# A three-stage kernel on one core: the TensorE order of the attention rounds, and two results in other PSUM banks

## What is computed

```python
for t in range(S):
    state = alpha[:, :, t, :, None] * state + np.einsum('bhd,bhe->bhde', k[:, :, t], v[:, :, t])
    y[:, :, t] = np.einsum('bhd,bhde->bhe', q[:, :, t], state)
```

## Time and profile before

| | us |
|---|---|
| median of 3 runs | 916.24 |
| lowest and highest | 914.87, 918.62 |
| the profiled execution, its own time | 919.07 |
| its span in the profile | 917.5 |
| PE busy | 881.7 (96% of the span) |
| DVE, ACT, POOL busy | 435.9, 320.4, 272.0 |
| attention rounds 0 to 15 | from 15.07 to about 187 of the span |

### The profile page before, as it was taken

How to read it: one execution, slowest core, us unless ns; L and a number is a source line. 1 busy time by engine, 2 the same in 40 slices (tenths; PEclk the granted TensorE clock), 3 DMA queues, 4 the chain that set the end, 5 groups by cost and what they waited for, 6 DMA issues and landing times. The chain is left out here.

```text
span 917.5 us, 16303 instructions
## 1 busy us (share of the span) xinstructions
PE 881.7 (96%) x5729; PEld 775.3 (85%) x5729; DVE 435.9 (48%) x826; ACT 320.4 (35%) x708; POOL 272.0 (30%) x279
## 2 busy tenths in 40 slices
PE   7999999888999999999998999999999999999995
PEld 5777787667899898998987899999999989999994
DVE  7777778782322223222234545445445445445442
ACT  4465646452322223222232233223223323223221
POOL 3113344545547544735807301001001001001001
PEclk9999999999999999999999999999999999999998
DMA  9886875768876897766806301001001002000000
GB/s 149 142 131 115 160 131 108 242 237 265 253 249 194 287 294 251 218 205 182 231 27 179 97 1 53 18 1 61 10 1 64 6 0 70 1 1 35 1 1 34
DMA packets 140975, 107.92 MB, mean 118 GB/s; under 512 B 103354, under 2 KB 129074, under 8 KB 140898
## 3 DMA queue, kind: packets, MB, share of 16 engines
q0 software_dynamic: 25696, 66.09, 22.9%
q1 hardware_dynamic: 115202, 40.79, 21.1%
HBM read 89.51 MB, written 17.35 MB: 116 GB/s over the span
## 5 line engine op out<-in xcount | busy, mean ns | idle before, releaser
L1396 POOL DMA_INDIRECT out<-of,idi x24 | 23.6, 983 | 370.2 <-DVE of L1482 305.5
L1216 PE MATMUL bank<-WX,hdTh 128*128 (+1 forms) x496 | 129.0, 341 | 3.6 <-issue 2.6
L1440 PE MATMUL bank<-xT_h,wi_h 128*128 128x512 f32 x288 | 114.1, 396 | 0.0
L1440 PE MATMUL bank<-xT_l,wi_h 128*128 128x512 f32 x288 | 113.6, 394 | 0.0
L1440 PE MATMUL bank<-xT_h,wi_l 128*128 128x512 f32 x288 | 113.4, 394 | 0.0
L1522 DVE TENSOR_SCALAR em<-ee 128x512 f32<-128x512 f32 x96 | 44.5, 464 | 136.3 <-ACT ee L1500 134.1
L1500 ACT ACTIVATE ee<-bank 128x512 f32<-128x512 f32 x96 | 57.3, 597 | 147.3 <-PE bank L1440 136.5
L1202 PE MATMUL bank<-WX,xdTh 128*128 (+1 forms) x372 | 99.7, 403 | 2.4 <-ACT xdTh L1242 1.3
L1503 ACT ACTIVATE g_h<-gg 128x512 fp32r<-128x512 f32 x96 | 60.6, 631 | 116.1 <-DVE gg L1527 114.4
L1140 POOL TENSOR_TENSOR WX<-raw_w,WX 128x3072 fp32r<-128x3072 f32 x14 | 95.6, 6829 | 17.6 <-DMA WX<-moe_w 13.2
L1531 DVE TENSOR_TENSOR g_l<-gg,g_h 128x512 fp32r<-128x512 f32 x96 | 69.7, 726 | 60.2 <-ACT g_h L1503 56.5
(11 more groups left out here) (212 smaller groups left out, 1392.8 us busy)
## 6 DMA issues: line engine op xcount, KB each, us to landing
WX<-moe_w POOLq DMA_DIRECT2D x14, 1536.0 KB, 10.1
raw_w<-moe_w POOLq DMA_DIRECT2D x14, 1536.0 KB, 7.8
xd<-sorted_x SPq DMA_DIRECT2D x31, 193.0 KB, 5.4
sorted_y<-yd SPq DMA_DIRECT2D x31, 192.5 KB, 4.0
xg<-sorted_y SPq DMA_DIRECT2D x6, 770.0 KB, 4.4
nat_a<-alpha SPq DMA_DIRECT2D x32, 144.0 KB, 3.2
nat_k<-k SPq DMA_DIRECT2D x32, 144.0 KB
nat_q<-q SPq DMA_DIRECT2D x32, 144.0 KB
```

Of the source, the lines that this page charges most:

```text
L1216: last = pe.matmul(y_out(t)[:, 0:DM], hdT[a][:, k * P:(k + 1) * P], WX[:, bass.ds(off + (b * WE + KD * F + k * DM), DM)], start=(k == 0 an ...
L1440: last = pe.matmul(bank[4 + i % 2][:, :], a[:, k, w], b[:, k, :], start=(k == 0 and m == 0), stop=(k == KD - 1 and m == 2))
```

## The change

In PE's table, `Yi0`, `Yi1`, `Ys0`, `Ys1` now stand together at the end of the round, so that both halves' logits with values run in one stretch and both halves' states with queries in the next. The transposes `Ta0`, `Ta1`, `Tq0`, `Tq1`, `Tk0` move ahead and are interleaved with `YN0` and `YN1`. To allow this, the second half of y goes to bank 6 instead of bank 7, and the increments of `KV` go to bank 5 instead of bank 6. So `YN0` now waits for `St5`, where it waited for `Kt1`. ACT's table changes with it: `yT0` and `yT1` are at the head of the next round around `Kt0`, and `Ea0` and `C1` come ahead of `Yn0`. `Rw` of the router, `Gq` of the last but one batch and one `SP` square move a few places, because bank 6 and the table changed.

```diff
-        ROUND_PE = (("KT0", 0), ("A0", 0), ("KT1", 0), ("Tk1", 1), ("KV", 0), ("A1", 0), ("YN0", -1), ("Ta0", 2), ("Yi0", 0),
-                    ("YN1", -1), ("Ta1", 2), ("Ys0", 0), ("Tq0", 1), ("Tq1", 1), ("Tk0", 2), ("Yi1", 0), ("Ys1", 0))
+        ROUND_PE = (("KT0", 0), ("A0", 0), ("KT1", 0), ("Tk1", 1), ("KV", 0), ("A1", 0), ("Ta0", 2), ("YN0", -1), ("Ta1", 2),
+                    ("Tq0", 1), ("YN1", -1), ("Tq1", 1), ("Tk0", 2), ("Yi0", 0), ("Yi1", 0), ("Ys0", 0), ("Ys1", 0))
-        ROUND_AC = (("yT1", -1), ("Kt0", 0), ("Kt1", 0), ("St1", 0), ("St2", 0), ("St3", 0), ("St4", 0), ("St5", 0),
-                    ("Yn0", -1), ("Ln0", -1), ("C1", 0), ("Ea0", 2), ("Yn1", -1), ("Ln1", -1), ("Ea1", 2), ("yT0", 0))
+        ROUND_AC = (("yT0", -1), ("Kt0", 0), ("yT1", -1), ("Kt1", 0), ("St1", 0), ("St2", 0), ("St3", 0), ("St4", 0), ("St5", 0),
+                    ("Ea0", 2), ("C1", 0), ("Yn0", -1), ("Ln0", -1), ("Ea1", 2), ("Yn1", -1), ("Ln1", -1))
...
         def y_bank(n, i):
-            return bank[1 if n == PAIRS - 1 and i else 7]
+            return bank[(1 if n == PAIRS - 1 else 6) if i else 7]
...
                             at_ = c % HC * P + DP * h
-                            last = pe.matmul(bank[6][DP * h:DP * h + DP, c * D:(c + 1) * D], ktsb[c // HC][:, at_:at_ + DP],
+                            last = pe.matmul(bank[5][DP * h:DP * h + DP, c * D:(c + 1) * D], ktsb[c // HC][:, at_:at_ + DP],
...
-                        acA.wait(pe, f"yT{1 - i}", n - 1 + i)
+                        acA.wait(pe, f"yT{i}", n - 1)
+                    for b in range(PARTIAL):
+                        if n == round_of(b, 1) and i:
+                            veA.wait(pe, "Rw", b)
...
-                        acA.wait(pe, "Kt1", n + 1)
+                        acA.wait(pe, "St5", n + 1)
...
-                    return ac.activation((st if i > 1 else std)[u][:, i, :], bank[6][:, (i - 1) * D:i * D], ACT.Copy,
+                    return ac.activation((st if i > 1 else std)[u][:, i, :], bank[5][:, (i - 1) * D:i * D], ACT.Copy,
```

More of the change, by code:

```diff
@@ L290, in build @@
                 {"R": ("Rp", "Rr"), "S5": ("Ng", "Nk"), "LA": ("Ns", "Nt", "Nr")})
-        SOON = ({"LA": ("Rl", "Rx", "Dl")}, {"R": ("Rc", "Rb", "Ro"), "F": ("Rs", "Rn", "Rd", "Y0"),
+        SOON = ({"LA": ("Rl", "Rx", "Dl")}, {"R": ("Rc", "Rb", "Ro"), "F": ("Rs", "Rn", "Rw", "Rd", "Y0"),
                                              "LA": ("Ng", "Nk", "Y1", "Y2", "Y3", "Y4", "Y5", "Y6", "Y7"),
-                                             "Qh1": ("Rw", "Rp", "Rr", "Ns", "Nt", "Nr")})
+                                             "Qh1": ("Rp", "Rr", "Ns", "Nt", "Nr")})
         LAST = ({"LA": ("Rl", "Rx", "Dl", "N0", "Rc", "Rb", "Ro", "Rs", "Rn", "Rd", "Rw", "Rp", "Rr", "Rz", "Ng", "Nk", "Ns", "Nt", "Nr",
@@ L297, in build @@
         ROUTE_PE = [({}, {"Ta0": ("CT",)})] * (BATCHES - 1) + [({"YN1": ("CT",)},)]
-        ROUTE_AC = [({}, {}, {"Ln0": ("Gq",)})] * (BATCHES - 2) + [({}, {"yT0": ("Gq",)}), ({"Ln1": ("SL", "Wc", "Gq")},)]
+        ROUTE_AC = [({}, {}, {"Ln0": ("Gq",)})] * (BATCHES - 2) + [({}, {"Ln1": ("Gq",)}), ({"Ln1": ("SL", "Wc", "Gq")},)]
         ROUTE_PO = [({"Zm": ("ID",)},)] * BATCHES
@@ L350, in steps_ac @@
                 i = place_of(out_, "St5") + 1
-                out_.insert(i, ("SP", PARTIAL * C + 2))
-                out_ += [("SM", PARTIAL)] + [("SP", PARTIAL * C + j) for j in range(3, C)]
+                out_[i:i] = [("SP", PARTIAL * C + j) for j in range(2, 4)]
+                out_ += [("SM", PARTIAL)] + [("SP", PARTIAL * C + j) for j in range(4, C)]
             for b, r in batches_of(n):
@@ L622, in step @@
                     acA.wait(pe, "St5", n - 1)
-                    for b in range(BATCHES):
-                        if n == round_of(b, 2):
-                            veA.wait(pe, "Rw", b)
                     for c in range(C - 1):
@@ L677, in step @@
                     veA.wait(pe, "Ro", n)
-                    acA.wait(pe, "St5", round_of(n, 1) if n < PARTIAL else PAIRS - 1)
+                    acA.wait(pe, "yT1", round_of(n, 0) if n < PARTIAL else PAIRS - 2)
                     for x, lhsT in enumerate((before, ones)):
```

## The result

The median went from 915.97 us (913.05 to 918.62) to 917.93 us (916.62 to 919.86), with 20 runs of each: a ratio of 1.0023, 95% interval 1.0013 to 1.0034, about +2 us. Forecast were +2.7 and "within 0.5%", and this is what came. The terms that make it up are not those of the forecast, though: that they add up to the right total is luck. The profiled execution of the changed kernel took 917.66 us (span 916.1).

What follows compares the result with a forecast made beforehand. PE was taken to set the pace of stage one. Terms -0.5 + 0.7 + 0.4 - 0.5 + 2.9 - 0.6 + 0.3 = +2.7 us on 916.2 gave 918.9 us; range from nearly 912 up to 923.5.

Steps and rivals of the forecast that it cites:

- Term 1: PE in each round: fewer changes of tiling, 0.64 us less work, 9 us over 14 full rounds if nothing waits.
- Term 2: Quiet rounds: YN1 waits 0.52 us for ACT's Ln0; round 10.19 against 10.31; rounds 2, 3, 4, 10 together -0.5.
- Term 3: Squares ahead of Yn0 on ACT delay YN1: +0.70 us in round 5, +0.4 in round 9; round 13 about -0.5.
- the formula: For rounds other than quiet ones: change in length equals the shift of YN1's start minus 0.38 us.
- Term 4: Late PE signals while POOL scatters: rounds 7, 8, 11, 12 +2.9 us, earlier scatters -0.6, rounds 14 and 15 +0.3.
- The clause on the bank: YN0's wait for St5, through a bank shared by address, costs nothing in quiet rounds, 2.2 us of standing in round 8.
- Round 6: ACT's table load now stands ahead of Ea1, for which Tk0 waits: 0 change, within 0.5 us.
- the scatter rounds pay little: Rival: late signals are out before St5 is wanted, four scatter rounds +0.1 each; about +0.8, 917 us; chance 0.20.
- the switches in full: Rival: Ln0 in time, each of 14 rounds gains PE's 0.64 us; -9, 907 us; chance 0.14.

Runs made afterwards that it cites:

- experiment 3: Changed kernel with ACT's Yn0 and Ln0 ahead of C1 and the two squares of rounds 5 and 9 at the round's end; 913.35 us, ratio 0.9956.
- experiment 5: Changed kernel with its last four PE steps ordered Yi0, Ys0, Yi1, Ys1, two more changes of tiling per round; 931.6 us, ratio 1.0089.
- experiment 6: Changed kernel with only ACT's Yn0 and Ln0 moved ahead of C1; 926.41 us, ratio 1.0051 to the kernel before.
- the kernel before, again: The kernel before, unedited, in a second execution under the profiler; 917.72 us.
- experiment 10: The kernel before with six matmuls of no use ahead of round 0, keeping PE busy; 915.01 us, ratio 0.9995; its profiled execution 914.59 us.
- experiment 7: Changed kernel with only the two squares of rounds 5 and 9 moved to the end of ACT's round; 924.67 us, ratio 1.0030.
- experiment 8: Changed kernel with the KV increments back in bank 6, so YN0 waits for Kt1, not St5; 926.25 us, ratio 1.0048.
- experiment 11: Changed kernel with Yn0, Ln0 ahead of C1 except round 14, squares at the end, Gq after Ln1, six matmuls ahead of round 0; 912.42 us, ratio 0.9969.
- experiment 4: Changed kernel with twelve matmuls nobody reads, six ahead of round 0 and six after the last YN1; 917.34 us, ratio 1.0004.

## Why the prediction was right, and where it was not

- **Term 1, mis-sized.** 0.64 us less PE work per round was forecast; the rows of experiment 3 give 0.44. I took `YN` for 0.67 where it follows transposes, without its 0.10 of coming in, since both use the whole array. It takes 0.75 (50.91 to 51.66) and 0.78 (52.40 to 53.18), together 0.19 too little. All other parts were right to 0.01 or 0.02 once the two short waits are taken out. So what costs is not the tiling alone; going from transposes to multiplying costs nearly as much with the tiling unchanged. Going back from `YN` to transposes costs nothing: the three of `Ta1` take 0.33 (52.19 to 52.52 in the changed kernel). Where the tiling did change, the price of 0.13 held (experiment 5). The Trainium skill (TensorEngine Tiling, Key Properties) speaks of changing the mode; this trace has a price between transposes and multiplying in one tiling too, 0.08 to 0.11 us on the way in.
- **Term 2, right in kind.** The wait is there for the reason given, at the time given (`YN1` at 6.13, forecast 6.09) and of nearly the size given (0.48 by starts, forecast 0.52), and it eats the whole gain. The round is 10.32 instead of 10.19 because `YN1` starts 0.04 later than forecast and takes 0.77 instead of 0.67. Experiments 3 and 6 confirm it: with `Yn0` ahead of `C1` quiet rounds are 10.09, 0.22 under the kernel before, and the rest of the 0.44 stays in the two short waits.
- **Term 3, right in kind, too small.** +0.95 in round 5 (forecast +0.70) and +0.95 in round 9 (forecast +0.4). `YN1` came at 7.27, where 7.28 was forecast. But the formula subtracted 0.38 for the work after it, and by rows that is 0.11 here (4.48 before, 4.37 after: 75.11 to 79.48) and 0.28 in a quiet round (4.20). So the step that was mis-sized is this 0.38. And the kernel before, again, has 10.69 in both rounds: the late mask of round 9 belonged to the first profile. Round 13 was forecast at -0.5, in part from the same mask, and changed by 0.01. The two rounds with squares are 1.90 of the +2.68 us.
- **Term 4, the wrong condition.** +2.9 - 0.6 + 0.3 was the largest part of the sum. In the profiles without late signals it is +0.04 for rounds 7, 8, 11 and 12 and +0.27 for round 14. It had been built on one profiled execution that was 3.1 us above the median, and the late signals alone were worth more than that (4.5 us, experiment 10). The mechanism was seen on another chip, in variants of the changed kernel, at about two thirds of the size (experiment 7), and with a consequence that the forecast lacked, falls of the clock at some of PE's longer waits. A near variant was 3.3 to 4.4 us slower than the kernel before there (experiment 8). How many of the 20 runs of either kernel had late signals is not known. The clause on the bank fell too: with the wait for `St5` taken away, round 8 has the same length (experiment 8).
- **Round 6**, put at 0 within 0.5, was +0.33: `Tk0` stands for `Ea1`, which comes behind the table load.

So the total came out by luck: term 4, too large by 2.3 in its four rounds (the 0.3 for rounds 14 and 15 came), stood against terms 2 and 3 and round 6, too small by 0.5, 1.3 and 0.3. Of the rivals, the second, "the scatter rounds pay little", names the actual condition; its +0.8 was too low for the same reasons. The third, the switches in full, needed a PE saving of 0.64, of which 0.44 is there, and an ACT order that the change does not have.

## What to carry to other kernels

When a better order on the bounding engine puts its waits closer together, look at once at the order of the engine that feeds it: here three copies and two squares stood ahead of the one result that PE wanted, and moving them gave some 5 us against the changed kernel (experiments 3 and 11), where the PE order alone had lost 2. Before a term is built on a wait in one profile, compare that execution's time with the median; a profile 3 us above it may hold something that most runs don't. A gain in a stage counts only if what starts the next stage, here scatters and a load, moves with it. And an edit that is to isolate a cause must not stand where its effect would show, as the six matmuls ahead of stage two did in experiment 4.

## What was not expected of the hardware

- PE's signals reach ACT up to 2.4 us after the matmuls end in rounds in which POOL issues scatters (`KV` done at 3.05, `St1` at 5.35; in experiment 8, round 11, 3.05 and 5.46), in some executions only: in all four profiles of one chip, in one of the two profiles of the result, and in none of eight on two other chips, with the same kernels or near ones. That the scatters hold them back is not shown. The kernel before was 6 to 7 us slower on the chip that shows them (922.93 against 915.76 to 916.75).
- In the changed kernel's first profile the granted clock is 0.50 from 14.4 to 17.8, after PE had waited 3.01 us for DVE's first scaled keys (to 13.13), and again for 3.4 us from 188.5. With six matmuls in that wait it stayed at 1.00 there in both orders, and round 0 of the changed kernel fell from 10.78 to 9.61; no change in the time of either kernel can be told.
- Going from transposes to multiplying in the same tiling costs PE nearly as much as entering another tiling, 0.1 us; going back costs nothing that the rows show.
- POOL's `M1` took 2.41 us in round 14 of experiment 3 and 0.87 in the changed kernel, with the same operands; PE then stood 1.20 us for it. In experiment 3 a scan of 1.75 us on DVE starts with it, at 167.34; whether that is the cause was not tried.
